# The token layer's output product is added by VectorE, straight from PSUM

## The reference

```python
scores = scale * q @ k.T
scores = where(scores >= max(scores) - tau, scores, -1e9)
x = softmax(scores) @ v                       # 4 batches x 8 heads, 576 x 64 -> (4, 576, 512)
h = relu(x.T @ w_tok1) @ w_tok2               # token layer, 256 hidden
u = x + h.T                                   # the addition that is changed
y = u + relu(u @ w_ch1) @ w_ch2               # channel layer, 1536 hidden
h = relu(y @ w_in)                            # then 3 taps over the tokens, sigmoid gate
out = (h * sigmoid(conv(h))) @ w_out
```

## Time and profile before

| | |
|---|---|
| median of three runs | 852.53 us |
| the profiled execution | 852.48 us |
| its span | 850.6 us |
| TensorE busy | 824.0 us (97%) |
| VectorE busy | 428.8 us (50%) |
| ScalarE busy | 410.6 us (48%) |
| GpSimd busy | 266.0 us (31%) |

### The profile page before, as it was taken

How to read it: one execution, slowest core, us unless ns; L and a number is a source line. 1 busy time by engine, 2 the same in 40 slices (tenths; PEclk the granted TensorE clock), 3 DMA queues, 4 the chain that set the end, 5 groups by cost and what they waited for, 6 DMA issues and landing times.

```text
span 850.6 us, 14725 instructions
## 1 busy us (share of the span) xinstructions
PE 824.0 (97%) x5512; PEld 654.9 (77%) x5512; DVE 428.8 (50%) x829; ACT 410.6 (48%) x866; POOL 266.0 (31%) x202
## 2 busy tenths in 40 slices
PE   7889999999999998899999999999999999999998
PEld 3556666666666666788888888888899989898996
DVE  6788888787878774601211211211213909156380
ACT  4787888877778775311211111211114737355461
POOL 0063324151423322480200100120290736528170
PEclk9999999999999999999999999999999999999999
DMA  9311111111111114000000000000320010100101
GB/s 265 116 57 51 50 52 49 49 49 49 49 49 49 49 18 149 1 1 1 0 1 1 1 0 1 1 1 0 124 76 1 2 51 1 42 21 0 49 0 62
DMA packets 20906, 33.75 MB, mean 40 GB/s; under 512 B 4416, under 2 KB 11136, under 8 KB 20864
## 3 DMA queue, kind: packets, MB, share of 16 engines
q1 hardware_dynamic: 20864, 33.18, 12.0%
HBM read 28.46 MB, written 4.72 MB: 39 GB/s over the span
## 4 chain that ended last, share of the span: by engine, by line
PE 88%; DVE 7%; issue 2%; ACT 2%; POOL 0%; DVEq 0%; ACTq 0%; POOLq 0%
PE score L1156 17%; PE score L1269 12%; PE score L991 6%; PE out_t L1171 4%; DVE prob L844 4%; PE turn_y L1171 4%; PE tails L1171 4%; PE mixed L1171 4%; PE out_t L1254 4%; PE out_t L1057 3%; PE mixed L1103 3%; PE mixed L1057 3%; PE score L1014 3%; PE turn_y L1254 3%; PE mixed L1254 3%; PE tails L1254 3%
## 5 line engine op out<-in xcount | busy, mean ns | idle before, releaser
L907 DVE SCALAR_TENSOR_TENSOR h<-score,h 128x512 fp32r<-128x512 f32 (+1 forms) x60 | 38.3, 638 | 243.0 <-ACT h L684 243.0
L684 ACT ACTIVATE h<-score 128x512 fp32r<-128x512 f32 (+1 forms) x60 | 33.3, 555 | 250.4 <-PE score L1156 250.4
L827 DVE TENSOR_SCALAR_CACHE_REDUCE negs<-score,neg_scale 128x576 f32<-128x576 f32 x144 | 112.7, 816 | 55.2 <-PE score L991 29.3
L844 DVE SCALAR_TENSOR_TENSOR prob<-negs,thresh,exps 128x576 f32<-128x576 f32 x144 | 140.3, 1006 | 0.3 <-ACT thresh L595 0.3
L592 ACT ACTIVATE exps<-negs,neg_max 128x576 f32<-128x576 f32 x144 | 104.7, 773 | 2.3 <-DVE negs L827 1.5
L1156 PE MATMUL score<-uh,w1h 128*128 128x512 f32 (+1 forms) x240 | 86.8, 368 | 0.0
L1156 PE MATMUL score<-uh,w1l 128*128 128x512 f32 (+1 forms) x240 | 86.8, 368 | 0.0
L1156 PE MATMUL score<-ul,w1h 128*128 128x512 f32 (+1 forms) x240 | 86.8, 368 | 0.0
L560 POOL TENSOR_TENSOR zl<-z,zh 128x512 fp32r<-128x512 f32 x32 | 54.2, 1695 | 99.0 <-ACT zh_t L765 99.0
L1014 PEld LDWEIGHTS score<-ident,prob 64*128 64x128 f32 x512 | 41.4, 139 | 44.3 <-issue 43.9
L991 PE MATMUL score<-qk 64*128 64x512 f32 x256 | 72.3, 641 | 0.0
(11 more groups left out here) (179 smaller groups left out, 2019.3 us busy)
## 6 DMA issues: line engine op xcount, KB each, us to landing
qk<-in_qk SPq DMA_DIRECT2D x16, 704.0 KB, 4.1
vm<-in_v SPq DMA_DIRECT2D x16, 320.0 KB, 4.3
result<-ostage SPq DMA_DIRECT2D x16, 256.0 KB, 2.1
w1f<-in_moe_w_ch SPq DMA_DIRECT2D x4, 768.0 KB, 11.0
w2f<-in_moe_w_ch SPq DMA_DIRECT2D x4, 768.0 KB, 8.2
wif<-in_moe_w_in SPq DMA_DIRECT2D x1, 2048.0 KB, 7.5
wof<-in_moe_w_out SPq DMA_DIRECT2D x8, 256.0 KB, 2.6
wt2f<-in_moe_w_tok SPq DMA_DIRECT2D x1, 576.0 KB, 9.8
```

The costliest lines, as they stand in the source:

```text
L827: nc.vector.tensor_scalar(negs[:, i, h, :], raw_of[h], neg_scale[:, 0:1], None, ALU.mult, ALU.min, accum_out=neg_max[:, i, h:h + 1]).then_ ...
L844: nc.vector.scalar_tensor_tensor(out=prob[:, i, h * S:(h + 1) * S], in0=negs[:, i, h, :], scalar=thresh[:, i, h:h + 1], in1=exps[i][:, h, ...
```

## The change

ScalarE's drain of the output product, GpSimd's addition, the buffer `u_part` and the semaphore `u_added` go. VectorE has an `add_u` of its own: for one half of a pair it waits for the product (and for x's two drains before the first half), reads the product from PSUM and x from SBUF, writes the sum over x and counts `u_drained`. Its places in VectorE's body are the head of steps 3 and 4 of an even pair (halves 0 and 1 of pair k - 4) and the head of step 0 of the odd pair after it (both halves of pair k - 4 as the odd body counts, the same that was made in step 4 before); the last pair's stands behind the last body. ScalarE waits for `u_drained` where it waited for `u_added`, and TensorE has one further wait in front of the fourth hidden tile.

```diff
             def body(at):                                   # GpSimd
                 g, k = at.g, at.k
-                if at.mix:
-                    add_u(g - 4)
                 for i in range(KT if at.hid else 0):
                     rest_of_token(at, i)
                 if at.pv:
                     split_x(at)
-                if at.mix:
-                    add_u(g - 3)
...
                     if s == 2:                              # ScalarE
-                        if at.mix:
-                            drain_u(g - 4, (0,))
...
-                        if at.mix:
-                            drain_u(g - 4, (1,))
...
-                        if at.mix:
-                            drain_u(g - 3)
...
-            act.wait_ge(u_added, PAIRS)
+            act.wait_ge(u_drained, 2 * PAIRS)
...
+            def add_u(pair, c):                             # VectorE
+                dve.wait_ge(u_done, 2 * pair + c + 1)
+                if c == 0:
+                    dve.wait_ge(xt_drained, pair + 1)
+                    dve.wait_ge(xt_tail_drained, pair + 1)
+                part = uy_pair[:, pair, c * HALF:(c + 1) * HALF]
+                nc.vector.tensor_tensor(part, (out_t, mixed)[c][:, 0:HALF], part, ALU.add).then_inc(u_drained, 1)
...
             def body(at):                                   # VectorE
                 for s in range(NT):
                     two, one = at.unit(s + 2), at.unit(s + 1)
+                    if s == 0 and at.k >= 5 and at.k % 2 == 1:
+                        for c in range(2):
+                            add_u(at.g - 4, c)
+                    if s >= 3 and at.mix:
+                        add_u(at.g - 4, s - 3)
                     if two:
                         copy_out(two)
...
             bodies(dve, body)
+            for c in range(2):
+                add_u(PAIRS - 1, c)
...
+                if n == EARLY - 1:                          # TensorE, hidden(n)
+                    pe.wait_ge(xt_tail_drained, PAIRS)
```

More of the change, by code:

```diff
@@ L137, in build @@
     h1f = s1.put("h1f", [P, KT, 2 * P])
-    u_part = s1.put("u_part", [P, S])
     h1h = s1.put("h1h", [P, KT, 2 * P], F32R)
@@ L254, in build @@
         u_done = sem("u_done")
-        u_added = sem("u_added")
         u_drained = sem("u_drained")
@@ L492, in rest_of_token @@
                     .then_inc(tok_lo, 1)
[L494 to L500, removed]
             def split_u(m):
@@ L656, in drain_x @@
                 nc.scalar.activation(uy_pair[:, pair, 0:MAIN], tails[:, :], ACT.Copy).then_inc(xt_drained, 1)
[L658 to L665, removed]
             def round_u(m):
@@ L696, in body @@
                     if s == 0 and k == PAIRS:
+                        act.wait_ge(u_drained, 2 * KM)
                         round_first_u(0)
```

## The result

The changed kernel takes 856.40 us in the median of five executions (855.80 to 856.72), the kernel before 852.53 us in five on the same chip: a ratio of 1.0045, 95% interval 1.0032 to 1.0058. It is slower by 3.9 us, where 5.0 us were forecast. The profiled execution of the changed kernel took 856.64 us, its span 854.8 us, 4.2 over that of before.

What follows compares the result with a forecast made beforehand. TensorE was taken to bound the kernel (88% of the chain). From 852.48 us, 6.5 lost at the join (pair 16's 0.4 included) less 1.5 gained in attention gave 857.5 us, range 855.2 to 860.6.

Steps and rivals of the forecast that it cites:

- attention: Even pairs in attention: masks end some 0.6 us earlier, removing five TensorE waits of 0.30 us, 1.5 us gained.
- pair 16: End of attention: TensorE's transposes of the attention output wait for VectorE's split of u and addition, 0.4 us lost.
- the rounds: VectorE's cast, subtract and rest of hidden tile for w2 at the join: 4.47 us each, two before the second projection.
- the clock: Rival, 15%: TensorE idle 5.0 us before the projections, its clock falls, costing 1.3 to 4.2 us; 860.2 us in all.
- Two signs: The prediction falls if projections start before 365 us, or attention up to the last scores moves by over 2 us.
- The join: From attention to the channel layer: w2 rounds queue behind the last additions, second projection 6.5 us later, pair 16 included.
- GpSimd out of the way: Rival, 15%: at the join the w2 rounds run without GpSimd's interference at 3.46 us each; 855.5 us in all.
- the six new waits of the products with v: Sign of being wrong: in odd pairs of attention, TensorE's products with v newly wait for VectorE's additions.
- the margin of 0.1 us: Odd pairs in attention: VectorE's two additions end some 0.1 us before the products with v need them.
- The additions bite: Rival, 14%: masks not earlier, TensorE waits for additions at each odd pair, 1.2 us lost in attention; 860.2 us.
- VectorE is the true bound: Rival, 3%: in attention all time masks lose beside GpSimd returns on the path, 12.6 us gained; 846.4 us.
- Taking turns: VectorE and GpSimd operations exclude each other for whole instructions; at the join the second projection starts 0.2 us later still.

Runs made afterwards that it cites:

- experiment 1: The kernel before, with VectorE's rounds of w2 held until the last output product is drained, nothing else of the change: 859.68 us, ratio 1.0083.
- experiment 2: The changed kernel with VectorE's four rounds of w2 moved ahead of body 18, before the additions of the last two pairs: 850.56 us, ratio 0.9987.
- experiment 4: The changed kernel with 20 useless 128x512 matmuls on TensorE filling the 4.7 us gap before the first projection: 855.68 us.
- experiment 5: The changed kernel with GpSimd's last five chunks of w1 held until VectorE has done all four rounds of w2: 855.51 us, ratio 1.0041.
- experiment 8: Experiment 2's kernel plus six filling matmuls and two VectorE reorders (u's split behind an addition, one addition ahead of the masks): 850.00 us, beside 849.98 without the reorders.

## Why the prediction was right, and where it was off

The direction, the place of the loss and its mechanism held: the w2 rounds stand behind a late product in VectorE's order, experiment 1 makes the loss without the rest of the change, and experiment 2 takes it out. The size came out near for a worse reason. In the profiled executions 4.2 us were lost, not 5.0: attention gave 1.3 more than its term (and the start-up 0.1), pair 16 cost 0.1 less and the rounds 0.5 less, and the clock, a rival and no term of the sum, took 1.2. That these errors partly cancel is luck.

Two signs that the prediction named as its own fall came. It was to fall if the projections started before 365 us; the first started at 362.42. And it was to fall if attention moved by more than 2 us; it moved by 2.8. Both have one cause, the gain of attention that it had too small: 362.42 is 2.7 us early by what was won ahead of it, and without that it would have been 365.1, just inside.

- *The join.* The chain was as forecast: last addition, first cast, round, round, with the second projection at its end. Its first cast came at 358.10; the forecast's 361.25, less its 0.4 for pair 16 and less the 2.7 in fact won ahead of the join, says 358.15. The first two rounds were 3.98 and 4.46 us, where twice 4.47 was taken: the first cast took 0.95 us as in the row that I used, but the first subtraction 2.48 in place of 2.97. Without the clock the second projection would have started at 366.65 (the next cast at 366.54 and 0.1), which makes 5.6 us from the last output product on, against 6.1 in the sum.
- *The clock*, a rival at 15%, came true: 1.2 us in the profiled execution, by experiment 4. The price I gave it was 1.3 to 4.2, and it came just under the lower end. The first projection took 5.26 us, not 5.74, and would have waited until 366.65 for the second round anyway, so its slowness cost 1.0 us (367.68); the clock was back early in the second projection, which cost 0.2 more.
- *GpSimd out of the way*, 15%, is refuted: it was in the way in both rounds, and without it rounds are 3.26 us (experiment 5).
- *Attention* was the mis-sized term: 2.8 us, not 1.5. The released transposes moved by 0.47 us and not by the 0.30 that the waits gave. The bracketed idle time counts from the modelled end of the matmul before; I take it that 0.17 us of the wait lay in that busy span. No run was made to test this, but experiment 8 fits: its brackets there are 0.06 us, and its transposes are 0.23 us behind those without any. The step of 0.14 us at the second output product had no bracket at all and was not in the sum. And the six new waits of the products with v, which the prediction had named as a sign against it, took 0.14 to 0.28 us back each; the margin of 0.1 us that the additions were to have was not there. Net 0.54 us per two pairs instead of 0.30.
- *Pair 16*: 0.28 us lost where 0.4 was taken (0.78 us of idle time in place of 0.50).
- *The additions bite*: TensorE did wait for the additions at each odd pair, but the masks were earlier too (0.5 us, seen from the matmuls around them), and the net is a gain. *VectorE is the true bound* is refuted: in 220 us of attention some 100 masks took 10 us less (mean 1.04 to 0.94 us), the additions there took 9, and the stage won 2.8 and not 12.6.
- *Taking turns*, which the Trainium skill (SBUF — State Buffer, Who interferes with whom) states and the prediction put beside the sum, fits the rows: GpSimd's operation ends at 362.65 + 1.75 = 364.40, 0.86 us into the subtraction that began at 363.54; 1.62 more make its 2.48 us, about the 1.76 that it takes alone. GpSimd's next, at 364.54, takes 2.61 us in place of 1.28. Its forecast for the join, 0.2 us more than the plain sum, was not better than the sum: the first cast did not wait, as GpSimd was at the end of an operation.

## What to carry to other kernels

When work is moved to an engine, look at what stands behind it in that engine's order: a wait for a late product, not the added work, made this change slow, though the engine was idle for 14 us in front of it. Idle time in brackets can be less than what a wait costs on TensorE (0.30 us stood for 0.47 here); compare the start of the same matmul. And a stop of TensorE can cost a second time through the clock: look at the granted clock of every execution, and fill the stop where nothing else can.

## What the runs showed of the hardware

- With a stop of TensorE of about 1.8 us before the join the granted clock fell in half of the executions (11 of 22); with 1.62 us in that place it fell in none of the 55 of the kernel before, and with the stop filled in none of 22. The executions of one kernel then differ by up to 4.4 us.
- VectorE's addition of 128x288 with one operand in PSUM took 0.44 to 0.46 us, as interpolated, and GpSimd's operations beside it did not lengthen it (0.46 at 357.72, with a conversion of w1 running); a mask of two SBUF operands went from 0.81 to 1.69 us.
